# Held-back loads, expert weights in four pieces and an earlier list of experts in a one-core attention, mixture-of-experts and mixing kernel

## Time and profile before

| | before |
|---|---|
| median of three runs | 430.6 us (429.65 to 431.72) |
| the profiled execution | 433.56 us, of it the span of the trace 431.1 us |
| PE busy | 412.0 us (96%) |
| DVE, ACT, POOL busy | 256.9, 195.4, 79.0 us |
| mean granted clock of PE | 0.992 of full speed |
| chain that ended last | PE 72%, DVE 7%, DMA 2% |

### The profile page before, as it was taken

One profiled execution on the slowest core, in us unless ns is written; L12 is line 12 of the kernel. 1 busy time (PEld: TensorE's weight loads), 2 busy tenths in 40 slices (PEclk: granted clock), 3 DMA queues, 4 the chain that ended last, 5 costly groups with the idle time before them and its releaser, 6 DMA issues.

```text
span 431.1 us, 8110 instructions
## 1 busy us (share of the span) xinstructions
PE 412.0 (96%) x2791; PEld 330.6 (77%) x2792; DVE 256.9 (60%) x427; ACT 195.4 (45%) x433; POOL 79.0 (18%) x127
## 2 busy tenths in 40 slices
PE   7869999999969999999999999999999999999997
PEld 3647787558858888888888778888888888888885
DVE  3885898899563714552216586566677555545352
ACT  1767997452455636473227574433343243123110
POOL 3684786221100111110030002500000000000000
PEclk9988999999999999999999999999999999999999
DMA  8999911161795341607240006500000000000012
GB/s 286 392 411 416 362 52 74 50 242 52 284 427 216 109 165 42 243 24 292 98 122 26 0 0 221 146 2 1 0 2 0 26 24 0 26 24 27 24 49 97
DMA packets 12942, 54.49 MB, mean 126 GB/s; under 512 B 1520, under 2 KB 1648, under 8 KB 11120
## 3 DMA queue, kind: packets, MB, share of 16 engines
q1 hardware_dynamic: 8080, 40.98, 24.5%
q0 software_dynamic: 2960, 9.70, 7.1%
q10 hardware_dynamic: 1872, 3.41, 2.0%
HBM read 40.46 MB, written 13.63 MB: 125 GB/s over the span
## 4 chain that ended last, share of the span: by engine, by line
PE 72%; DVE 7%; DMA 2%; ACT 1%; issue 1%; DVEq 1%; ACTq 0%; SPq 0%; POOL 0%
PE ps L1536 13%; PE ps L1538 13%; PE ps L1537 13%; PE ps L1684 8%; PE ps L1686 8%; PE ps L1685 8%; PE ps L1622 2%; PE ps L1558 2%; DMA w_raw<-w 2%; DVE w_l L1068 2%; PE ps L1591 2%; PE ps L1577 1%; PE ps L1531 1%; ACT w_h L731 1%; PE ps L1404 1%
## 5 line engine op out<-in xcount | busy, mean ns | idle before, releaser
L1684 PE MATMUL ps<-z_h,mix_h 128*128 128x512 f32 x144 | 56.9, 395 | 0.0
L1686 PE MATMUL ps<-z_h,mix_l 128*128 128x512 f32 x144 | 56.1, 390 | 0.0
L1685 PE MATMUL ps<-z_l,mix_h 128*128 128x512 f32 x144 | 56.1, 390 | 0.0
L1536 PE MATMUL ps<-w_h,hT_h 128*128 128x512 f32 x104 | 42.0, 403 | 2.6 <-DVE hT_l L1092 2.0
L1068 DVE TENSOR_TENSOR w_l<-w_raw,w_h (+1 forms) x32 | 37.4, 1219 | 10.4 <-ACT w_h L731 10.4
L680 ACT ACTIVATE p<-s,nmax 128x120 f32<-128x120 f32 x96 | 36.5, 385 | 11.9 <-DVE nmax L913 11.9
L1538 PE MATMUL ps<-w_l,hT_h 128*128 128x512 f32 x104 | 40.7, 391 | 0.0
L1537 PE MATMUL ps<-w_h,hT_l 128*128 128x512 f32 x104 | 40.6, 390 | 0.0
L1536 PE MATMUL ps<-w_h,xT_h 128*128 128x512 f32 x96 | 38.5, 401 | 1.5 <-DVE w_l L1068 1.5
L1538 PE MATMUL ps<-w_l,xT_h 128*128 128x512 f32 x96 | 37.4, 390 | 0.0
L1537 PE MATMUL ps<-w_h,xT_l 128*128 128x512 f32 x96 | 37.4, 390 | 0.0
(11 more groups left out here) (264 smaller groups left out, 863.3 us busy)
## 6 DMA issues: line engine op xcount, KB each, us to landing
w_raw<-w SPq DMA_DIRECT2D x8, 2048.0 KB, 10.5
mix_raw<-mix SPq DMA_DIRECT2D x2, 2304.0 KB, 13.5
ys<-zero SPq DMA_DIRECT2D x1, 3840.0 KB, 37.6
kfull<-k_full SPq DMA_DIRECT2D x8, 400.0 KB, 9.2
vpad<-v_pad SPq DMA_DIRECT2D x4, 768.0 KB, 12.4
xd<-x_sb POOLq DMA_DIRECT2D x12, 256.0 KB, 2.3
ys<-y_sb ACTq DMA_DIRECT2D x12, 256.0 KB, 2.1
out<-o SPq DMA_DIRECT2D x12, 256.0 KB, 2.0
```

The costliest lines, as they stand in the source:

```text
L1536: pe.matmul(ps[:, bank, :], a_h[:, k, :], w_h[:, n, :], start=(k == 0), stop=False)
L1684: pe.matmul(ps[:, i, :], w_h, zh, start=(jb == 0 and m == 0), stop=False)
L1685: pe.matmul(ps[:, i, :], w_h, zl, start=False, stop=False)
L1686: mm = pe.matmul(ps[:, i, :], w_l, zh, start=False, stop=(jb == TPB - 1 and m == 1))
```

## The change

- SP's queue no longer issues all loads at once. The values wait for the second pair of keys, the keys of batch 1 for the first half of the values, the last queries for `norm_done` of tile 0, expert 0's w1 for tile 1, its w2 for tile 3, and the zeros, now in two DMAs, for tiles 5 and 7. Queries come in DMAs of two tiles (4 KB rows).
- Each w1 or w2 load comes as four DMAs with 4 KB rows, each with its own semaphore; ACT waits for each of the four steps by itself, written out without a hardware loop. The halves of the mixing matrices come as three DMAs with 6 KB rows each, and the second half waits until expert 1's w2 has landed.
- `list_experts` writes the experts before the gather counts; a new semaphore `after_ready` tells of the counts, and SP waits for it only ahead of the w2 load. The list has its own buffers.
- In the attention PE turns tile 1's exponentials before it makes the scores of tile 3; ACT copies `pT` of tile 1 before the exponentials of tile 2; the second half of `pT` goes to DVE for tiles 0 and 1; the key maxima of batch 1 are taken two in tile 1 and two in tile 2.
- Five warm-up matmuls instead of six at the start, and one warm-up matmul more ahead of the last tile's logits.
- Five semaphores of the first routing step become one that counts. Waits on `raw_in` and `zeros_in` count the new DMAs.

```diff
@@ -37,8 +37,9 @@
 EARLY = NU // 2 // PER
+MIX = 3
 assert PER * UNITS == NU and UNITS < NS_MIN - 2 and F == SW * DM
-WARM, WARM_SUM, WARM_SLOTS = (6, 1), (1, 0), (3, 1, 1, 1)
+WARM, WARM_SUM, WARM_SLOTS = (5, 1), (1, 0), (3, 1, 1, 1)
 MAGIC = 1.5 * 2.0 ** 23
@@ -442,8 +449,13 @@
         def _(sp):
+            def load_weights(raw, src, arrived):
+                for i in range(STEPS):
+                    sp.dma_start(raw[:, i * SW:(i + 1) * SW, :], src[:, i * SW:(i + 1) * SW, :]).then_inc(arrived[i], 16)
+
             def load_q(n):
-                sp.dma_start(q_all[:, Q_PARTS[n]:Q_PARTS[n + 1]], q_d[:, Q_PARTS[n]:Q_PARTS[n + 1]]).then_inc(q_in[n], 16)
+                for g in range(Q_PARTS[n], Q_PARTS[n + 1], 2):
+                    sp.dma_start(q_all[:, g:g + 2], q_d[:, g:g + 2]).then_inc(q_in[n], 16)
 
@@ -458,44 +470,56 @@
             sp.dma_start(const[:, 0:C_UT], const_d[:, 0:C_UT]).then_inc(const_in, 16)
+            sp.wait_ge(kfull_in[0][1], 16)
             load_v(0)
...
             load_q(1)
+            sp.wait_ge(v_in[0][0], 16)
             load_keys(1)
             load_v(1)
+            sp.wait_ge(norm_done, 1)
             load_q(2)
             sp.dma_start(const[:, C_UT:C_END], const_d[:, C_UT:C_END]).then_inc(rconst_in, 16)
-            sp.dma_start(w1_raw[:, :, :], w1_d[0]).then_inc(w1_in, 16)
-            sp.dma_start(w2_raw[:, :, :], w2_d[0]).then_inc(w2_in, 16)
+            sp.wait_ge(norm_done, 2)
+            load_weights(w1_raw, w1_d[0], w1_in)
+            sp.wait_ge(norm_done, 4)
+            load_weights(w2_raw, w2_d[0], w2_in)
             sp.wait_ge(zeroed, 1)
-            sp.dma_start(ys_t[TPB:NS].rearrange("t p n -> p t n"),
-                         zero[:, :].unsqueeze(1).broadcast_to([P, NS - TPB, DM])).then_inc(zeros_in, 16)
+            for i in range(2):
+                sp.wait_ge(norm_done, TPB + 2 * i)
+                part = slice(TPB + i * (NS - TPB) // 2, TPB + (i + 1) * (NS - TPB) // 2)
+                sp.dma_start(ys_t[part].rearrange("t p n -> p t n"),
+                             zero[:, :].unsqueeze(1).broadcast_to([P, part.stop - part.start, DM])).then_inc(zeros_in, 16)
 
...
             def load_mix(i):
-                part = slice(i * NU // 2, (i + 1) * NU // 2)
-                sp.dma_start(mix_raw[:, part, :], mix_d[:, part, :]).then_inc(raw_in[i], 16)
+                for n in range(i * NU // 2, (i + 1) * NU // 2, MIX):
+                    sp.dma_start(mix_raw[:, n:n + MIX, :], mix_d[:, n:n + MIX, :]).then_inc(raw_in[i], 16)
 
...
                 e = sp.value_load(table[0:1, X_EXPERT, bass.ds(p, 1)], min_val=0, max_val=E - 1)
-                sp.wait_ge(w1_in, p * 16)
+                for i in range(STEPS):
+                    sp.wait_ge(w1_in[i], p * 16)
                 sp.wait_ge(w1_split, p * STEPS + STEPS)
                 sp.sem_inc(passed_sp, 1)
-                sp.dma_start(w1_raw[:, :, :], w1_d[bass.ds(e, 1)].rearrange("o p n d -> (o p) n d")).then_inc(w1_in, 16)
+                load_weights(w1_raw, w1_d[bass.ds(e, 1)].rearrange("o p n d -> (o p) n d"), w1_in)
+                sp.wait_ge(after_ready, 1)
                 gathers = sp.value_load(table[0:1, X_AFTER, bass.ds(p, 1)], min_val=1, max_val=NS - 3)
-                sp.wait_ge(w2_in, p * 16)
+                for i in range(STEPS):
+                    sp.wait_ge(w2_in[i], p * 16)
                 sp.wait_ge(w2_split, p * STEPS + STEPS)
...
                 sp.sem_inc(passed_sp, 1)
-                sp.dma_start(w2_raw[:, :, :], w2_d[bass.ds(e, 1)].rearrange("o p n d -> (o p) n d")).then_inc(w2_in, 16)
+                load_weights(w2_raw, w2_d[bass.ds(e, 1)].rearrange("o p n d -> (o p) n d"), w2_in)
 
...
             load_expert(1)
+            sp.wait_ge(w2_in[STEPS - 1], 32)
             load_mix(1)
@@ -693,11 +717,13 @@
             def tile(g, s, ex=True):
+                if g == 1:
+                    pT_copy(g)
                 if ex:
                     exps(g + 1, 1 - s, range(0, H // 2))
-                if g != NT - 2:
+                if g not in (1, NT - 2):
                     pT_copy(g)
-                if g <= SUMMARY_TILES:
+                if 1 < g <= SUMMARY_TILES:
                     pT_copy(g, 1)
@@ -707,8 +733,7 @@
             exps(1, 1, range(0, H // 2), first=True)
-            for u in range(2):
-                pT_copy(0, u)
+            pT_copy(0, 0)
             exps(1, 1, range(H // 2, H), first=True)
@@ -725,10 +750,9 @@
                 with act.If(new != 0):
-                    act.wait_ge(arrived, (place + 1) * 16)
-                    act.sem_inc(passed_act, 1)
-                    with act.Fori(a, b) as i:
-                        act.activation(hi[:, bass.ds(i * SW, SW), :], raw[:, bass.ds(i * SW, SW), :], ACT.Copy).then_inc(done, 1)
+                    for i in range(a, b):
+                        act.wait_ge(arrived[i], (place + 1) * 16)
+                        act.activation(hi[:, i * SW:(i + 1) * SW, :], raw[:, i * SW:(i + 1) * SW, :], ACT.Copy).then_inc(done, 1)
 
@@ -756,14 +780,14 @@
             act.wait_ge(scores_ready, NT)
-            act.wait_ge(w1_in, 16)
             for i in range(STEPS):
+                act.wait_ge(w1_in[i], 16)
                 act.activation(w1_h[:, i * SW:(i + 1) * SW, :], w1_raw[:, i * SW:(i + 1) * SW, :], ACT.Copy).then_inc(w1_hi, 1)
...
             act.wait_ge(av_ready, NT)
-            act.wait_ge(w2_in, 16)
             for i in range(STEPS):
+                act.wait_ge(w2_in[i], 16)
                 act.activation(w2_h[:, i * SW:(i + 1) * SW, :], w2_raw[:, i * SW:(i + 1) * SW, :], ACT.Copy).then_inc(w2_hi, 1)
@@ -943,6 +967,8 @@
                     first_keys()
+                if g <= 1:
+                    pT_copy(g, 1)
                 if g + 2 < NT:
@@ -1050,7 +1076,7 @@
                 tile(g, g % 2)
-                key_summary(1, {0: [0], 1: [1, 2], 2: [3]}.get(g, []))
+                key_summary(1, {1: [0, 1], 2: [2, 3]}.get(g, []))
             lg_copy(NT - 2)
@@ -1198,16 +1224,16 @@
                 tiles = r_te[:, :, :].rearrange("p t v -> p (t v)").rearrange("p (v t) -> p v t", t=NS)
+                link(dve.scalar_tensor_tensor(r_ord[:, E:V], r_used[:, E:V], r_last[:, 1:2], r_ord[:, E:V], ALU.add, ALU.subtract))
+                link(dve.tensor_tensor(r_xe[:, :, :], r_ord[:, :].unsqueeze(1).broadcast_to([1, V, V]),
+                                       const[0:1, C_TILE:C_TILE + V].unsqueeze(2).broadcast_to([1, V, V]), ALU.is_le))
+                link(dve.tensor_reduce(out=r_xs[:, :], in_=r_xe[:, :, :], op=ALU.add, axis=AX))
+                link(dve.tensor_scalar(r_xf[:, :], r_xs[:, :], -1.0, V - 1.0, ALU.mult, ALU.add))
+                dve.tensor_tensor(table[0:1, X_EXPERT, 0:V], r_xf[:, :], r_xs[:, :], ALU.min).then_inc(experts_ready, 1)
                 link(dve.scalar_tensor_tensor(tiles, r_tf[:, :].unsqueeze(1).broadcast_to([1, V, NS]), 2.0,
...
                 link(dve.tensor_reduce(out=r_start[:, 0:V], in_=tiles, op=ALU.add, axis=AX))
-                link(dve.tensor_scalar(table[0:1, X_AFTER, 0:V], r_start[:, 0:V], 1.0, r_n3[:, :], ALU.add, ALU.min))
-                link(dve.scalar_tensor_tensor(r_ord[:, E:V], r_used[:, E:V], r_last[:, 1:2], r_ord[:, E:V], ALU.add, ALU.subtract))
-                link(dve.tensor_tensor(r_te[:, 0:V, :], r_ord[:, :].unsqueeze(1).broadcast_to([1, V, V]),
-                                       const[0:1, C_TILE:C_TILE + V].unsqueeze(2).broadcast_to([1, V, V]), ALU.is_le))
-                link(dve.tensor_reduce(out=r_start[:, 0:V], in_=r_te[:, 0:V, :], op=ALU.add, axis=AX))
-                link(dve.tensor_scalar(r_tf[:, 0:V], r_start[:, 0:V], -1.0, V - 1.0, ALU.mult, ALU.add))
-                dve.tensor_tensor(table[0:1, X_EXPERT, 0:V], r_tf[:, 0:V], r_start[:, 0:V], ALU.min).then_inc(experts_ready, 1)
+                dve.tensor_scalar(table[0:1, X_AFTER, 0:V], r_start[:, 0:V], 1.0, r_n3[:, :], ALU.add, ALU.min).then_inc(after_ready, 1)
 
@@ -1364,7 +1390,8 @@
                 if g in Q_PARTS:
-                    pe.wait_ge(q_in[Q_PARTS.index(g)], 16)
+                    n = Q_PARTS.index(g)
+                    pe.wait_ge(q_in[n], (Q_PARTS[n + 1] - g) // 2 * 16)
                 pe.wait_ge(kw_set, g + 1)
@@ -1451,10 +1483,10 @@
 
-                if sc and not first:
+                if sc and g > 1:
                     scores(g + 2, s)
                 transpose_p(g, s, first)
-                if first:
+                if g <= 1:
                     scores(g + 2, s)
@@ -1492,6 +1524,7 @@
             sum_logits(NT - 2)
+            keep_warm(1)
             route_logits(NT - 1)
@@ -1584,7 +1612,8 @@
             routing_ranks()
-            pe.wait_ge(w1_in, 16)
+            for i in range(STEPS):
+                pe.wait_ge(w1_in[i], 16)
             pe.wait_ge(xTf_taken, 1)
```

More of the change, by code:

```diff
@@ L188, in program @@
         r_ord = sb("r_ord", [1, V])
+        r_xe = sb("r_xe", [1, V, V])
+        r_xs = sb("r_xs", [1, V])
```

(40 more changed lines are left out.)

## The result

The changed kernel takes **427.41 us** (median of 6 runs, 426.71 to 428.45) against 430.85 us (429.65 to 432.05, 6 runs) of the kernel before, run beside it: ratio 0.9922, 95% interval 0.9898 to 0.9946. It is 3.4 us faster; 421.5 us, 9.1 us faster, was forecast. The profiled execution took 426.71 us, its span 424.8 us.

A forecast was written before the change was run, and what follows sets the result against it. PE was taken as the bound from about 130 us, ACT in the attention's steady part; 5.3 + 0.3 + 0.4 + 2.8 + 0.3 = 9.1 us off the median 430.6 gave 421.5 us, range 418.5 to 428.0 us.

The forecast's parts named there:

- Loads held back: Attention, 25 to 40 us: holding loads brings PE's late code fetch in time, ending gap and half clock; 5.3 us gained.
- The fetch stays late: Rival, attention: busy DMA engines still delay the code fetch, so 5.3 us stay lost; 426.8 us, chance 0.27.
- A second dry page: Rival, attention: another code fetch falls into w1's or w2's burst, a second loss of 5.3 us; 432.1 us, chance 0.09.
- signs of being right: Attention: no PE "issue" gap over 1 us before 50 us; from 25 to 40 us full clock, ACT busy over 4 of 5.
- Four pieces, and the earlier list: Expert 1: w1 issued 1.3 us earlier and landing in pieces shortens PE's waits of 1.5 and 2.0 us; 2.8 us gained.
- Loops written out: Last expert's w2: ACT's steps without loops cut PE's 0.7 us loss; 0.3 us gained.
- Less between in the first loads: Kernel start: values issued later leave engines to keys, queries and constants for the first scores; 0.3 us gained.
- Tile 1's turn: Attention's first tiles: tile 1's turn first, copies moved from ACT to DVE; 0.4 us gained, bounds -0.5 and 1.0 us.
- No cost: Warm-up matmuls at start and ahead of last logits, counting semaphore and more SP waits were claimed to cost nothing.

The follow-up runs named there:

- e10: Kernel before with only the list of experts written ahead of the gather counts, weights whole; 429.74 against 431.29 us, ratio 0.9954.
- e11: Kernel before with later experts' weights in four pieces and ACT's steps written out, list of experts late; 429.91 us, ratio 0.9953.
- e5: Kernel before with one extra warm-up matmul ahead of the last logits, nothing else; 430.68 against 430.5 us, ratio 0.9995.
- e2: Kernel before with the middle alone: expert loads in four pieces, early list, second mixing half behind expert 1's w2; 427.58 us, ratio 0.9905.
- e1: Kernel before, unchanged, run and traced again; median 432.15 against 431.46 us, ratio 1.0001.
- e9: Changed kernel with first w1 and w2 later in halves, zeros in five stores, and the middle as before; 428.89 us, ratio 0.9931 to the kernel before.
- e3: Changed kernel with its middle undone: whole expert loads, late list, no wait ahead of the second mixing half; 432.18 us, ratio 1.0008 to the kernel before.
- e6: Kernel before with tile 1's turn first, pT copies moved to DVE, batch 1's key maxima in tiles 1 and 2; 431.37 us, ratio 1.0005.
- e13: Kernel before with two waits only: first w1 at norm_done 4, w2 and the whole zeros at norm_done 6; 432.03 against 430.64 us, ratio 1.0039.
- e7: Kernel before with only the first loads held back, queries and first weights in pieces, zeros in two held stores; 432.64 against 430.5 us, ratio 1.0041.
- e14: Changed kernel with first weights later in halves, zeros in five stores, without holds on values, batch 1's keys and last queries; 424.19 us, ratio 0.9858 to before.
- e4: Changed kernel with the two stores of zeros moved out of the attention, behind the first mixing half; 430.56 us, ratio 0.9993 to the kernel before.
- e8: Changed kernel with first w1 in halves at norm_done 4 and 5, w2 at 6 and 7, zeros in five stores; 424.65 us, ratio 0.9870 to before.
- e12: Changed kernel with only first w1 and w2 later in halves, zeros in two stores right behind; 425.18 us, ratio 0.9837 to the kernel before.

## Why the prediction was wrong

**"Loads held back", 5.3 us, is the step that failed**, in three ways.

*It was sized on an unusual execution and taken from the median.* e10 and e11 have the attention of before untouched, with a gap of 1.3 to 1.4 us and a full clock, and their mark is at 75.8 to 76.0 us. The trace that I read has it at 79.8. The other traces of this attention have it at 75.7 (e5, with the extra matmul), 76.2 (e2) and 78.2 us (e1). Some 4 of the 5.3 us were therefore missing in four of these five traces, and 1.6 us in e1. What is left is small: with every gap gone (e9) the whole attention side gives 2.4 us, not the 6.0 of the forecast. The 106 runs of before in the four sessions (one more, at 643.5 us, is left out) show what a median holds: 30 with a mean clock of 0.999 or more took 429.3 us in the median, 51 at 0.995 to 0.996 431.2, 19 at 0.991 to 0.992 433.1, and 6 at or under 0.988 435.3. Each step of 0.004 goes with one more short fall of the clock and 1.9 to 2.2 us: e2 and e5 at 0.996 have one in their traces, e3, e6 and e13 at 0.992 have two. The profiled one had 0.992, for one fall that lasted twice as long; the median one had 0.996. I noted the 3.0 us between it and the median and moved the starting point by them, but took the full term off all the same. Most of the 3.0 was in all likelihood the term itself: behind the mark the trace is ordinary (351.3 us, e9 351.4).

*The hold does not make room for the code.* In e7 the same gap of 2.69 us stands at the same place. The shorter queue and rows, on which I argued, did not take it away; a lower DMA share did (0.18 in e14 and 0.17 in e13 at 30 to 35 us, and no gap there). The change issues w1 at 25.27 us, which keeps the share at 1.02 up to 35 us, and its packet of code starts at 32.75 us, 187 matmuls behind the one before. In e14 w1 is issued at 36.71 us; the packet starts at 30.25 us, 112 matmuls behind, and PE never waits. I had named this outcome and given it 0.27. The Trainium skill, "DMA: Bandwidth & Descriptors", section "Queues, rings and completion order", has each DMA engine take turns between queues, packet by packet. The trace of e7 agrees as far as it goes: holding the queue short did not bring the code sooner.

*The held zeros bring a second gap.* e4 takes it away by moving them (mark 1.3 us earlier). Where the clock was full up to the mark, the attention of the change ends at 77.0 us, that of before at 75.7 to 76.2 (e2, e5, e10, e11): the hold costs some 1 us. Among executions with a full clock e7 is at 431.1 us (5 runs) and before, beside it, at 429.3 us (15 runs), which agrees in sign; e7's interval over all runs starts just above no change.

**What came true of the rivals.** "The fetch stays late" (426.8 us) is the outcome, 0.6 us off, and only by this rival does the measured time lie in the stated range. That it comes so near is in part luck: this rival had neither the 1 us that the hold costs nor the clock falls that it saves, and the two about cancel. "A second dry page" came true as well, not in the burst of w1 or w2 but in that of the zeros, and, in the profiled execution, at 1.7 us without a fall of the clock rather than 5.3 us (in e7 and e13 the clock fell behind it to 0.66). I priced both as if a gap always brought the half clock. Of the signs of being right, the full clock came; the gaps of over 1 us and ACT's 3.8 to 3.9 of 5 us did not fit.

**"Four pieces, and the earlier list" (2.8) and "Loops written out" (0.3)** held, 3.1 us against 3.5 us of rest (351.3 to 347.8). Both waits and the 0.5 us left at the last expert's w2 came as forecast to 0.2 us: ACT starts 3.2 us earlier (2.7 to 3.1), hT_l keeps 0.3 us (0.5). The split was off: in its trace the list by itself gives 0.8 us, not 1.3, since the wait for the hidden values then keeps its 1.9 us; the pieces by themselves give 3.2 of 3.5 us. I had not seen a second gain. In five of the eight traces with both waits in place (e3, e5, e6, e7, e13, but not before, e1 and e9) the clock fell right behind them; here e5's stretch:

```profile
121.70:125.70 4.00, 1.93 (x11) 1.45 (x10) 2.45 (x8) 1.62 (x3) 1.15 (x2) 1.00 1.00 409
125.70:129.70 4.00, 4.00 (x12) 3.10 (x12) 2.12 (x4) 2.13 (x4) 0.00 (x0) 0.58 0.95 400
```

PE works 1.93 of 4 us, then runs at 0.58. Their rest is 1.4 to 1.7 us longer than the 351.3 us of before (3.1 in e6, which has a second fall behind the mark). In none of the seven traces with the pieces did it fall there.

**"Less between in the first loads", 0.3 us**: e14 shows none of it. **"Tile 1's turn", 0.4 us**: e6 says between 1.3 us faster and 1.7 us slower; its size is not settled. One slip in the working: a tile takes 4.0 us there and 4.2 us in DVE's share, which by the same sum would make DVE's turn 3.4 instead of 3.6 us and the first term 5.7 instead of 5.3 us. **"No cost"** held as far as these runs can tell; whether the extra warm-up matmul pays is open.

**The sum, by measured terms.** Between executions with a full clock: middle -3.5, attention +1.2 (77.0 against 75.8), so -2.3 us; the runs give -1.9 us, 427.4 us (three of the change at 0.999 or more) against 429.3 us. The other 1 to 1.5 us of the 3.4 would be falls of the clock that come less often or cost less: the three runs of the change at 0.995 to 0.996 have a median of 427.9 us, against 431.2 us of before. That share is an estimate by subtraction from few runs; no run forces a fall.

## What to carry over

Before a gap in one trace is subtracted from a median, look whether the trace's mean clock is that of the median run, and take a second trace of the same kernel: here three quarters of the largest term (4 of 5.3 us) were not in most other traces of the same attention. In this kernel a load that nobody needed soon was best issued after PE's next code had come, and in pieces with room between (e8, e12, e14); holding it back by less, or issuing two together behind the wait (e13), only moved the full stretch. Waits of 1.5 to 2 us close together on PE can cost more than themselves, for the clock fell behind them in five of eight traces, for 1.4 to 1.7 us more.

## What the runs showed of the hardware

PE goes on 2.3 to 2.6 us after its late packet of code starts, in each of the pairs: 27.75 and 30.29 us (before), 32.75 and 35.08, 53.88 and 56.40 (changed), 57.69 and 60.06 (e12). That queue q8 carries PE's code is my reading of this match and of the matmuls between packets; no run shows it directly. The Trainium skill, "Runtime: NRT & Kernel Launch", section "Instruction fetch mechanics", calls the crossing of a block of code mostly hidden. Most of the packets here cost PE nothing either; with the DMA engines full when one is due, some cost it 0.4 to 2.7 us.

The clock falls from 2.4 to 1.2 GHz behind the same idle time in one execution and not in the next: after a gap of 1.50 us at 35 us it fell to 0.66 of full speed in e3 (35 to 40 us), and after gaps of 1.49 us there it stayed full in e4 and e6. One fall cost 1.7 us (4.52 against 2.82 us for six matmuls, e1).

Full engines are not enough for a large gap. In the first trace of before the DMA share is 0.98 to 1.06 from 35 to 50 us, and PE's largest "issue" gap there is 0.62 us; e12's DMA share is 1.00 and 0.99 from 50 to 60 us and it loses 0.45 us there; e14 has 0.97 from 50 to 55 us and loses nothing, while e13 loses 2.07 us. What decides which fetch is late by how much is not settled.
